# A fused attention and two-MLP kernel: two q tiles and one tile's v windows moved ahead of batch 0's v block rows in the load queue

## The chip, the cores and the metric

The kernel runs on one core of a Trainium2 chip. The metric is device time in microseconds (us), the median of a few runs. TensorE is written PE below (PEld is its weight load), VectorE is DVE, ScalarE is ACT, GpSimd is POOL, and SyncE, which issues almost all loads, is SP (SPq in rows of its queue).

## The reference

For two batches of eight heads, 768 rows and a head width of 64, the reference computes an attention in which every row sees the keys less than 16 rows away and, beside them, one summary key and one summary value for each block of 32 rows (the maximum of the block's keys, the mean of its values). Two MLPs follow on the 1536 x 512 result.

```python
k_sum = k.reshape(B, H, nb, block, D).max(axis=3)
v_sum = v.reshape(B, H, nb, block, D).mean(axis=3)
...
scores_all = np.concatenate([scores_l_m, scores_s], axis=-1)
...
v_all = np.concatenate([v, v_sum], axis=2)
return np.matmul(a, v_all).astype(np.float32)
...
silu = g * (1.0 / (1.0 + np.exp(-g)))
return (silu * val @ w_out).astype(np.float32)
...
h = x @ w_in
g = h - np.tanh(h)
return (g @ w_out).astype(np.float32)
```

## The kernel before

Each engine has one instruction stream written by hand; semaphores tie them together. Nothing is scheduled by a planner, so each engine works strictly in its written order.

Attention goes in tiles of 128 rows, six tiles (0 to 5) for batch 0 and six for batch 1. Batch 0 is done first. For a tile t the loads are: `kn` (the keys, 256 KB), `qn_a` (the queries, 256 KB, three buffers), and `vw_a` (the values, two overlapping windows of 96 rows, 192 KB each, three buffers). Beside them stand the block rows `blk`: all values of a batch, arranged as 96 partitions by 2 halves by 2048 numbers, from which the summary values are made. They are loaded in two halves of 768 KB each (`load_block_half`, L222). Their view of v in DRAM has four groups of heads outermost.

How batch 0 starts: PE transposes the six k tiles and q's tile 0 (`transpose_k`, L444; `transpose_q`, L460), ACT copies them back, DVE takes the block maxima of k (L1003), and PE computes tile 0's scores (`scores`, L485). DVE's written order then is `reduce_half(0)`, `reduce_half(1)`, `shift(A0, 0, 0, ...)`. The two halves are the sums over each block of v (L995, each waits for its half of `blk`); `shift` (L1016) is the step without which ACT cannot take tile 0's exponentials (L799). PE's order is `scores(A0, 0)`, `transpose_q(A0, 1)`, `summary_values` (L530, waits for both halves' sums), six small products that do nothing but keep PE occupied (L646), then the transposes of tile 0's probabilities (L500), tile 1's scores, tile 2's q transpose, and the products of probabilities and values (`weigh_values`, L521).

What comes next in the load queue also depends on that chain: tile 3's value windows reuse tile 0's buffer, so SP waits for `pv_done`, which PE gives at the end of tile 0's second `weigh_values`. Only behind that wait does SP issue batch 1's two halves of `blk`:

```python
for t in range(3, TPB):
    if t == 3:
        load_q0(4)
    load_v0(t)
    if t == 3:
        load_q0(5)
        for hf in range(2):
            load_block_half(1, hf)
    load_k(TPB + t)
```

Batch 1's block rows are added up on POOL (`add_halves`, L388). POOL's first such step stands in its order ahead of `inverse_rms` of tile 2 (L373, L376), which DVE's `scale_x` (L1049), PE's `transpose_x` (L537) and all that follows wait for. After batch 0's attention the MLPs begin (L543 to L545), interleaved with batch 1's attention, and run to the end.

Of the kernel before, what the change touches and what calls it, by code (L numbers as in the profile page):

```python
# [6 lines left out]
def attention_then_two_mlps(nc: bass.Bass, q, k, v, moe_w_gate, moe_w_val, moe_w_out, moe_rms_g,  # L7
# [58 lines left out]
    with ctx:  # L66
# [150 lines left out]
        def _(sp):  # L217
            def load_block_half(g, hf):

                if g:  # L220
                    sp.wait_ge(blk_red, hf + 1)
                sp.dma_start(blk[:, hf, :], v_b[g, hf]).then_inc(blk_in[hf], 16)  # L222

            def load_k(t):

                if t >= TPB:
                    sp.wait_ge(k_T, t - TPB + 1)
                sp.dma_start(kn[t % TPB][:, :].rearrange("p (h d) -> p h d", h=H),  # L228
                             k_v[t // TPB, t % TPB * P:(t % TPB + 1) * P]).then_inc(kn_in[t % TPB], 16)

            def load_windows(dst, src, t, done):
                for w in range(2):
                    sp.dma_start(dst[0:WIN, w, :].rearrange("p (h d) -> p h d", h=H),
                                 src[rows(window_start(t, w), WIN)]).then_inc(done, 16)

            def load_q0(t):
                if t >= 3:
                    sp.wait_ge(q_T, t - 2)
                sp.dma_start(A0.qn[t % 3][:, :].rearrange("p (h d) -> p h d", h=H),
                             q_v[0, t * P:(t + 1) * P]).then_inc(q_in[t % 3], 16)  # L240

            def load_v0(t):
                if t >= 3:
                    sp.wait_ge(pv_done, 2 * (t - 3) + 2)
                load_windows(A0.vw[t % 3], v_v[0], t, vw_in[t % 3])
# [38 lines left out]
            load_q0(0)  # L284
            for t in range(3, TPB):
                load_k(t)
            for hf in range(2):
                load_block_half(0, hf)
            load_q0(1)
            load_v0(0)  # L290
            load_v0(1)
            with nc.allow_non_contiguous_dma(reason="512 single elements, once"):
                sp.dma_start(rms_g[:, :], g_v).then_inc(g_in, 16)
            load_q0(2)
            load_v0(2)
            load_q0(3)
            for t in range(TPB, TPB + 3):
# [693 lines left out]
        def _(dve):  # L991
# [60 lines left out]
            def xT_low(t, src):  # L1052
                dve.wait_ge(xT_hi_done, t + 1)
                (dst, t0), (high, _) = place(xT_lo, t), place(xT_hi, t)
                for c in range(KC):
                    last = nc.vector.scalar_tensor_tensor(  # L1056
                        out=dst[:, c, rows(t0, P)], in0=src[:, c * P:(c + 1) * P], scalar=rms_g[:, c:c + 1],
                        in1=high[:, c, rows(t0, P)].bitcast(f32), op0=ALU.mult, op1=ALU.subtract)
                last.then_inc(xT_lo_done, 1)
# [211 lines left out]
```

## Time and profile before

| what | value |
|---|---|
| time, median of 3 runs | 694.68 us (694.16 to 695.09) |
| span of the profiled execution | 692.5 us |
| time outside the span (median less span) | 2.2 us |
| PE busy | 648.3 us, 94% of the span |
| DVE, ACT, POOL busy | 331.9, 271.8, 31.9 us |
| queue of SP's loads | 49.82 MB |

The time of the profiled execution itself is given only by its span; the span stands 2.2 us under the median of the unprofiled runs, and that difference is taken to lie around the span. A share of busy time is an average over the whole span. The first part, up to about 90 us, is attention with PE often idle, and the rest is the MLPs.

### The profile page before, as it was taken

What the parts mean: (1) busy time and instruction counts of PE and PEld (TensorE: products, weight loads), DVE (VectorE), ACT (ScalarE), POOL (GpSimd) and SP (SyncE); (2) the same over time, 40 slices, a digit from 0 to 9 for tenths busy, and PEclk for the clock granted to TensorE, in tenths of its full rate; (3) what the DMA queues carried; (4) which work ended last, traced back from release to release, by engine and by line L of the source; (5) the groups of instructions that cost most, each with busy time, mean ns of one, the idle gap of its engine ahead of it and who ended that gap; (6) DMA issues with size and microseconds to landing.
All of it is one profiled execution on the core that took longest, in us unless ns stands there. A gap on an engine that the chain in (4) does not pass through costs nothing.

```text
span 692.5 us, 11670 instructions
## 1 busy us (share of the span) xinstructions
PE 648.3 (94%) x4176; PEld 606.3 (88%) x4176; DVE 331.9 (48%) x754; ACT 271.8 (39%) x677; POOL 31.9 (5%) x66
## 2 busy tenths in 40 slices
PE   7273699999999999999999999999999999999997
PEld 7162589999999999999989999999999999989886
DVE  2573775676675323444444445555521254444442
ACT  3184554556454223333333333333311143333332
POOL 2012410001100000000000000000000000000000
PEclk9598799999999999999999999999999999999999
DMA  7674723313431212222222242222203022122202
GB/s 157 139 151 130 180 62 79 75 49 95 98 90 41 61 54 69 72 69 68 65 61 61 61 137 62 67 73 72 76 24 99 1 65 71 62 61 61 61 15 91
DMA packets 105852, 53.34 MB, mean 77 GB/s; under 512 B 46560, under 2 KB 99808, under 8 KB 105440
## 3 DMA queue, kind: packets, MB, share of 16 engines
q1 hardware_dynamic: 104096, 49.82, 27.4%
q10 hardware_dynamic: 1728, 3.15, 1.2%
q8 instruction: 18, 0.29, 0.2%
q14 instruction: 10, 0.08, 0.0%
HBM read 49.81 MB, written 3.15 MB: 76 GB/s over the span
## 4 chain that ended last, share of the span: by engine, by line
PE 85%; DMA 6%; DVE 3%; ACT 2%; SPq 1%; issue 1%; POOL 1%; DVEq 0%; ACTq 0%; POOLq 0%
PE bank L543 20%; PE bank L545 20%; PE bank L544 20%; PE bank L636 6%; PE bank L637 6%; PE bank L635 6%; DMA blk<-in_v_dram 6%; PE bank L521 1%; PE bank L500 1%; SPq L228 1%; ACT xT_hi L817 1%; ACT pr_b L799 1%; POOL blk L388 1%; DVE xT_lo L1056 1%; PE bank L485 1%
## 5 line engine op out<-in xcount | busy, mean ns | idle before, releaser
L543 PE MATMUL bank<-xT_hi,x_hi 128*128 128x384 f32 x448 | 151.6, 338 | 0.6 <-DVE xT_lo L1056 0.6
L545 PE MATMUL bank<-xT_hi,x_lo 128*128 128x384 f32 x448 | 150.2, 335 | 0.0
L544 PE MATMUL bank<-xT_lo,x_hi 128*128 128x384 f32 x448 | 150.2, 335 | 0.0
L1063 DVE TENSOR_TENSOR h_lo<-pd,h_hi 128x384 fp32r<-128x384 f32 (+1 forms) x112 | 62.9, 561 | 70.4 <-ACT h_hi L872 37.1
L543 PEld LDWEIGHTS bank<-xT_hi,x_hi 128*128 128x128 f32 x448 | 84.1, 188 | 3.3 <-DVE xT_lo L1056 0.9
L544 PEld LDWEIGHTS bank<-xT_lo,x_hi 128*128 128x128 f32 x448 | 84.1, 188 | 1.4
L545 PEld LDWEIGHTS bank<-xT_hi,x_lo 128*128 128x128 f32 x448 | 84.1, 188 | 0.0
L637 PE MATMUL bank<-y_hi,h_lo 128*128 128x512 f32 x192 | 76.0, 396 | 0.0
L636 PE MATMUL bank<-y_lo,h_hi 128*128 128x512 f32 x192 | 76.0, 396 | 0.0
L635 PE MATMUL bank<-y_hi,h_hi 128*128 128x512 f32 x192 | 75.9, 395 | 0.0
L1063 DVE TENSOR_TENSOR y_lo<-y_raw,y_hi 128x512 fp32r<-128x512 f32 x56 | 38.5, 688 | 77.3 <-ACT y_hi L832 77.3
L543 PE MATMUL bank<-xT_hi,y_hi 128*128 128x384 f32 x192 | 66.0, 344 | 0.0
L543 PE MATMUL bank<-h_hi,z_hi 128*128 128x384 f32 x192 | 65.2, 340 | 0.0
L544 PE MATMUL bank<-h_lo,z_hi 128*128 128x384 f32 x192 | 65.0, 339 | 0.0
L545 PE MATMUL bank<-h_hi,z_lo 128*128 128x384 f32 x192 | 65.0, 339 | 0.0
L832 ACT CAST y_hi<-y_raw 128x512 fp32r<-128x512 f32 x56 | 34.8, 621 | 75.5 <-PE bank L637 75.5
L545 PE MATMUL bank<-xT_hi,y_lo 128*128 128x384 f32 x192 | 64.3, 335 | 0.0
L544 PE MATMUL bank<-xT_lo,y_hi 128*128 128x384 f32 x192 | 64.2, 334 | 0.0
L856 ACT CAST h_hi<-pd 128x384 f32 (+1 forms) x48 | 24.7, 515 | 94.3 <-DVE pd L1092 94.1
L1118 DVE TENSOR_TENSOR pd<-bank,th 128x384 f32<-128x384 f32 x64 | 35.6, 557 | 30.4 <-ACT th L870 30.4
L872 ACT CAST h_hi<-pd 128x384 fp32r<-128x384 f32 x64 | 32.8, 513 | 40.7 <-DVE pd L1118 40.7
L870 ACT ACTIVATE th<-bank 128x384 f32<-128x384 f32 x64 | 31.4, 491 | 40.8 <-PE bank L545 40.8
(102 smaller groups left out, 903.6 us busy)
## 6 DMA issues: line engine op xcount, KB each, us to landing
x_raw<-in_moe_w_in_dram SPq DMA_DIRECT2D x32, 256.0 KB, 3.0
y_raw<-in_moe_w_out_dram SPq DMA_DIRECT2D x32, 256.0 KB, 2.7
x_raw<-in_moe_w_gate_dram SPq DMA_DIRECT2D x24, 256.0 KB, 3.0
y_raw<-in_moe_w_val_dram SPq DMA_DIRECT2D x24, 256.0 KB, 3.3
z_raw<-in_moe_w_out_dram SPq DMA_DIRECT2D x16, 384.0 KB, 3.4
kn<-in_k_dram SPq DMA_DIRECT2D x12, 256.0 KB, 5.1
blk<-in_v_dram SPq DMA_DIRECT2D x4, 768.0 KB
out_dram<-stage ACTq DMA_DIRECT2D x12, 256.0 KB, 2.5
```

Source lines behind the costliest of these rows:

```text
L543: nc.tensor.matmul(dst, w_hi, a_hi, start=start, stop=False)
L544: nc.tensor.matmul(dst, w_hi, a_lo, start=False, stop=False)
L545: return nc.tensor.matmul(dst, w_lo, a_hi, start=False, stop=stop)
L635: nc.tensor.matmul(AB[t][:], a_hi, w_hi, start=first, stop=False, skip_group_check=True)
L636: nc.tensor.matmul(AB[t][:], a_hi, w_lo, start=False, stop=False, skip_group_check=True)
L637: last = nc.tensor.matmul(AB[t][:], a_lo, w_hi, start=False, stop=final, skip_group_check=True)
L832: nc.scalar.copy(y_hi[:, s, :, :], y_raw[:, s, :, :]).then_inc(y_hi_done, 1)
L856: nc.scalar.copy(dst, pd[:, b, :]).then_inc(h_hi_done, 1)
L870: nc.scalar.activation(th[:, b, :], XB[b][:, 0:NB], ACT.Tanh).then_inc(tanh_done, 1)
L872: nc.scalar.copy(h2_hi[:, s, b, :], pd[:, b, :]).then_inc(h_hi_done, 1)
L1063: nc.vector.tensor_tensor(dst, full, high.bitcast(f32), ALU.subtract).then_inc(done, 1)
L1118: nc.vector.tensor_tensor(pd[:, b, :], XB[b][:, 0:NB], th[:, b, :], ALU.subtract).then_inc(x_bank_free, 1)
```

## The change

Only the order in which SP issues loads at the start changes. q's tile 1, the two windows of v's tile 0 and q's tile 2 were issued behind the two halves of `blk` (q's tile 2 further back still, behind v's tile 1 and the norm weights `rms_g`); they are now issued ahead of them. No load is added, removed or resized, no wait is added, and PE, DVE, ACT and POOL have the same instructions in the same order.

```diff
             load_q0(0)
             for t in range(3, TPB):
                 load_k(t)
+            load_q0(1)
+            load_v0(0)
+            load_q0(2)
             for hf in range(2):
                 load_block_half(0, hf)
-            load_q0(1)
-            load_v0(0)
             load_v0(1)
             with nc.allow_non_contiguous_dma(reason="512 single elements, once"):
                 sp.dma_start(rms_g[:, :], g_v).then_inc(g_in, 16)
-            load_q0(2)
             load_v0(2)
             load_q0(3)
```

This is SP's queue at the start of the program, before. Each row is a run of equal DMA issues, with the tile, its source and the shape.

```order
L239 DMA qn_a<-in_q_dram 128x8x64
L228 DMA kn<-in_k_dram 128x8x64 x3
L222 DMA blk<-in_v_dram 96x1x2048 x2
L239 DMA qn_a<-in_q_dram 128x8x64
L233 DMA vw_a<-in_v_dram 96x8x64 x4
L293 DMA rms_g<-in_moe_rms_g_dram 128x4x1
L239 DMA qn_a<-in_q_dram 128x8x64
L233 DMA vw_a<-in_v_dram 96x8x64 x2
L239 DMA qn_a<-in_q_dram 128x8x64
```

The same place of SP's queue in the changed kernel (one line more in the source moves `rms_g` to L294):

```order
L239 DMA qn_a<-in_q_dram 128x8x64
L228 DMA kn<-in_k_dram 128x8x64 x3
L239 DMA qn_a<-in_q_dram 128x8x64
L233 DMA vw_a<-in_v_dram 96x8x64 x2
L239 DMA qn_a<-in_q_dram 128x8x64
L222 DMA blk<-in_v_dram 96x1x2048 x2
L233 DMA vw_a<-in_v_dram 96x8x64 x2
L294 DMA rms_g<-in_moe_rms_g_dram 128x4x1
L233 DMA vw_a<-in_v_dram 96x8x64 x2
L239 DMA qn_a<-in_q_dram 128x8x64
```

Four more DMAs, 896 KB in all, now stand ahead of the two `blk` halves, and four fewer behind them. Among themselves the moved loads keep their order, and so do those that stayed behind `blk`.

## Rows read from the trace of the kernel before

**Rows 1.** The page: span, TensorE's busy slices, granted clock (40 slices, tenths).

```profile
span 692.5 us, 11670 instructions
...
PE   7273699999999999999999999999999999999997
...
PEclk9598799999999999999999999999999999999999
```

**Rows 2.** Chain that ended last, 0 to 120 us: start, us, what.

```profile
7.34 1.00 SPq L222
8.39 19.51 DMA blk<-in_v_dram
27.93 3.60 DVE redv L995
31.58 1.90 PE bank L530 x8
...
42.63 0.64 PE bank L521 x16
...
44.99 0.98 SPq L222
46.02 19.07 DMA blk<-in_v_dram
65.34 4.47 POOL blk L388
...
73.55 1.09 PE bank L537 x4
```

**Rows 3.** Timeline of DVE, 14 to 35 us; brackets: idle before, and releaser.

```profile
19.56 3.57 DVE L995 TENSOR_REDUCE redv<-blk 96x64 f32<-96x2048 f32 x1 [6.01 <-DMA blk<-in_v_dram]
27.93 3.59 DVE L995 TENSOR_REDUCE redv<-blk 96x64 f32<-96x2048 f32 x1 [4.80 <-DMA blk<-in_v_dram]
31.45 0.27 DVE L1016 CUSTOM_DVE_ANT_0 neg_a<-bank,mask 128x120 f32<-128x120 f32 x1
```

**Rows 4.** Timeline of SP's queue, start and length of the issues.

```profile
9.08 0.47 SPq L239 DMA_DIRECT2D qn_a<-in_q_dram  x1
9.59 19.29 SPq L233 DMA_DIRECT2D vw_a<-in_v_dram  x4
...
30.39 1.85 SPq L233 DMA_DIRECT2D vw_a<-in_v_dram  x2
...
37.30 1.14 SPq L239 DMA_DIRECT2D qn_a<-in_q_dram  x1
```

**Rows 5.** Stretches of 1 us; last columns: clock, DMA share, GB/s.

```profile
5.00:6.00 1.00, 1.00 (x12) 1.00 (x11) 0.00 (x0) 0.00 (x0) 0.66 (x3) 1.00 1.33 235
...
7.00:8.00 1.00, 1.00 (x12) 1.00 (x11) 0.00 (x0) 0.39 (x1) 0.09 (x1) 1.00 1.35 217
...
19.00:20.00 1.00, 0.00 (x0) 0.00 (x0) 0.44 (x1) 0.00 (x0) 0.00 (x0) 0.50 0.26 106
...
34.00:35.00 1.00, 1.00 (x6) 1.00 (x6) 0.00 (x0) 1.00 (x6) 0.00 (x0) 0.50 1.33 171
```

**Rows 6.** Waits up to 110 us (first row); timeline of PE (second row).

```profile
PE bank L460 <- DMA qn_a<-in_q_dram: 14.1, 1, 14.1
```

```profile
29.27 1.09 PE L460 MATMUL bank<-ident,qn_a 128*128 128x128 f32 x4 [14.14 <-DMA qn_a<-in_q_dram]
```

**Rows 7.** Stretches of 0.5 us, columns as in rows 5.

```profile
35.00:35.50 0.50, 0.50 (x6) 0.50 (x5) 0.00 (x0) 0.50 (x4) 0.00 (x0) 0.93 1.38 182
...
72.50:73.00 0.50, 0.00 (x0) 0.00 (x0) 0.50 (x1) 0.00 (x0) 0.50 (x1) 0.50 1.19 323
...
79.00:79.50 0.50, 0.50 (x14) 0.50 (x14) 0.50 (x2) 0.50 (x4) 0.00 (x0) 0.55 0.97 281
```

**Rows 8.** Timeline of PE: the same transposes at full and at half clock.

```profile
54.94 0.65 PE L500 MATMUL bank<-ident,pr_a 128*120 128x128 f32 x4
...
77.72 1.11 PE L500 MATMUL bank<-ident,pr_a 128*120 128x128 f32 x4
```

## The prediction

> **What bounds the kernel now.** I read the page first. PE is busy in nine tenths or more of every slice from the sixth on but the last, and only the first five (87 us) show gaps [rows 1]. So a change in the order of the first loads can act only on those roughly 90 us; afterwards PE has its fixed work, and whatever the start gains or loses arrives at the end unchanged.
>
> Next the chain of work that ended last [rows 2]. The reader is to see two long DMA pieces in it, both `blk`. The first begins with SP's issue at 7.34 us and ends when the second half has landed at 27.9. DVE sums that half in 3.60 us, and at 31.58 PE starts the summary products. From there the chain runs through compute until the end of tile 0's `weigh_values` (42.63 plus 0.64). That releases SP, which issues batch 1's `blk` at 44.99 and 46.0; it lands 19.07 us later. POOL, DVE and PE follow it, and PE is at work again at 73.55. So batch 0's `blk` is on the path, and batch 1's `blk` hangs on it through `pv_done`.
>
> The timeline of DVE shows that nothing can slip around the first piece [rows 3]. DVE sits idle 6.01 us and then 4.80 us, both times for `blk`, and the first `shift` starts at 31.45, right behind the second sum. DVE works in its written order, so `shift` cannot start ahead of the sums, whenever its scores were ready. The waits name one more: PE waited 14.1 us for q's tile 1, until 29.27 [rows 6]. That is the wait which the change addresses. Behind it in PE's order stand the summary products, which could not have started before 31.5 anyway, since they need DVE's second sum. Transposing q's tile 1 takes 1.09 us at the low clock, from 29.27 to 30.36, and leaves 1.2 us of idle time before 31.58 [rows 2, 6]. The wait is real and worth nothing.
>
> Then the DMA side. From 5 to 10 us the channels carry 217 to 235 GB/s (k's last tiles, in 256-byte rows). From 13 to 24 us, while only `blk` moves, they carry about 106 GB/s at a mean busy share of 0.26, against 1.33 before [rows 5]; of eleven rows one stands there, and the others lie within 98 to 115 GB/s. A share of 0.26 of sixteen channels is four channels' worth. So `blk` runs at 1,573 kB / 106 GB/s = 14.8 us for both halves, on about four channels that are full, while the others idle. SP's queue says what lies behind them: q's tile 1 was issued at 9.08 and landed at 29.2, just behind `blk`, and the next issue, v's first window, was held at SP; four window issues took 19.29 us [rows 4]. Loads pass through `blk`'s channels in the order of issue. What is issued ahead of `blk` therefore delays it, by the time those channels need for their share.
>
> **The change part by part.** *Four loads go ahead of blk.* They are 2 x 256 KB of q and 2 x 192 KB of v, 917.5 kB in all. They spread over all the channels as the k tiles do, in the same 256-byte rows, and the queue is full at this point, so their price is time at the saturated rate. By bytes: 917.5 kB at the 217 to 235 GB/s of the k tiles is 4.2 to 3.9 us. By SP's issue time with a full queue: a q tile takes 1.14 us, a pair of v windows 1.85 [rows 4], together 2 x 1.14 + 1.85 = 4.1 us. The two ways agree, and I take 4.1. The bounds come from the fastest and slowest stretch with mixed loads: 323 GB/s gives 2.8 us, 171 GB/s gives 5.4 [rows 5, 7]. Zero is excluded, since those four channels must carry their part of 917.5 kB before they turn to `blk`.
>
> Here a rule of the Trainium skill speaks for a smaller price. The page "DMA: Bandwidth & Descriptors", section Specifications, gives about 358 GB/s as a core's limit from HBM, by which the four loads would be an estimated 2.6 us; the same table says that rows under 512 B do not reach line rate. The trace agrees with the second: these rows are 256 B, and the k loads run at 217 to 235 GB/s [rows 5]. The sum by the first would be 2.6 in place of 4.1.
>
> *blk lands later.* The first half (19.56 us before) would be summed from about 23.7; the sum takes 3.57 us and is over well before the second half, so it stays covered. The second half lands at 27.9 + 4.1 = 32.0, the sum ends at 35.6, and shift, exponentials and summary products all start 4.1 us later. What of that is covered? DVE, PE and ACT have all been idle for `blk`, so nothing.
>
> *What is earlier.* q's tile 1 is transposed and copied at about 13 to 15 us. This takes 1.09 us of PE and an ACT copy out of a place where both were idle: gain 0. v's tile 0 and q's tile 2 are there in time before as well; PE shows no DMA wait other than that one of 14.1 us in the stretch. Gain 0.
>
> *What is later next.* v's tile 1, `rms_g`, v's tile 2, q's tile 3 and batch 1's first three k tiles are issued behind `blk`, as before. Before, the held issues ended at 28.88 and SP finished q's tile 4 at 37.30 + 1.14 = 38.44, then waited until 43.3 for PE [rows 2, 4]. That is 4.8 us of cover. Everything up to there moves by the same 4.1 as `pv_done`, and one q tile less is in it, so the cover stays. If it were gone, batch 1's `blk` would be issued later by what is missing; even both v windows of tile 1 held until `blk` has landed cost only 1.85 of the 4.8.
>
> *Batch 1.* `pv_done` comes at 43.3 + 4.1 = 47.4, and batch 1's `blk`, 19.07 us from issue to landing, lands at 69.2 in place of 65.1. Ahead of it stand the same loads as before (two windows, one q tile), and its own 14.8 us do not change. POOL, DVE, PE follow without slack, PE waiting for them before 73.55. Added here: nothing.
>
> *Sum.* 692.5 + 4.1 = 696.6 us of span; with the 2.2 us outside it, 698.8 us, which is 694.68 + 4.1.
>
> **The clock.** PE's granted clock is 0.50 (1.2 GHz) after the idle time before 29 us and comes back to 1.00 (2.4 GHz) within 35.0 to 35.5, at 0.93 over that stretch, 3.5 us after the summary products began at 31.58. In the second such place work began at 73.55 and the clock was back only in 79.0 to 79.5, 5.9 us later [rows 2, 7]. Before, q's transposes at 29.27 preceded the products; now there is no PE work between about 15 and 35.7 us. If the clock took 5.9 us to return in place of 3.5, 2.4 us of PE work would run at half speed and lose 1.2 us (four transposes take 1.11 in place of 0.65 [rows 8]). I put it at 0 in the sum and keep 1.2 as its upper end.
>
> **The rivals.** *A, the forecast:* the whole chain moves by the time of four loads, 698.8; its own range is 697.5 (2.8 us) to 700.1 (5.4 us). Chance 0.74.
>
> *B, the clock comes back late as well:* 4.1 + 1.2 gives 700.0. For it speaks that PE now starts cold with no work ahead; against it, that the work just ahead of the products was only 1.09 us with a gap behind it. Chance 0.14.
>
> *C, the delay is hidden:* the moved loads pass mostly on the channels that `blk` leaves idle, or the chain behind has slack that the profile does not show, and the time is within 1.4 us of before, about 695.2. For it speaks that twelve channels' worth stands idle from 13 to 24 us; against it, that q's tile 1 landed only behind `blk`, so a part of each load does use `blk`'s channels [rows 4, 6]. Chance 0.08.
>
> *D, faster:* what `blk` suffers from is sharing, and not order. Its halves landed 8.37 us apart (19.56, 27.93) [rows 3], against 7.42 for one half at 106 GB/s. If the v windows let in behind it slowed it, and the four loads cost it nothing, each half would gain 0.95: the place is the landing at 27.9, the price -1.9 us, the time 692.8. It decides only if the four loads cost under 1.9 us, which needs over 480 GB/s where the highest stretch has 323. Chance 0.04.
>
> **How the numbers follow.** A measurement of this kernel can tell about 0.2%, 1.4 us. A and B are slower by more, 0.88 together, of which I leave 0.02 for a price under 1.4 us: slower 0.86. C, with that 0.02, is 0.10 within. D is 0.04 faster. The range takes in A's bounds and B, and widens A's low end slightly for a second half that no longer shares: 697.2 to 701.2. It leaves out C, D and the tails of A and B, somewhat under 2 in 10.
>
> **What would show it.** In the profile of the changed kernel the DVE sum of the second half should start near 32.0 with idle time for `blk` ahead of it, the first `shift` near 35.6, and q's tile 1 transposed by 15 us with its 14.1 us wait gone. `weigh_values` of tile 0 should end near 47.4, batch 1's `blk` be issued near 49.1 and land near 69.2, still about 19 us. The span should be near 696.6. Wrong would be: a second sum that starts under 30 us (rival C or D), a clock that rises later than 3.5 us behind the summary products (B), or `blk` of batch 1 no longer 19 us from issue to landing.

## The result and the profile after

| kernel | median, us | runs | ratio to before, 95% interval |
|---|---|---|---|
| before | 694.85 (694.16 to 695.09) | 4 | |
| changed | 699.05 (698.68 to 699.5) | 4 | 1.0062 (1.0048 to 1.0076) |

The change costs 4.2 us; by the interval it is 3.3 to 5.3. (One run more of the kernel before than in the table of the start moves its median from 694.68 to 694.85.) The profiled execution of the changed kernel took 699.23 us, with a span of 697.4, 4.9 above that of before [rows 1]. In the four runs of the changed kernel the time stands 1.78 to 1.86 us above the span. With the same difference the profiled execution of the kernel before took about 694.3 (an estimate, 692.5 plus 1.8): it was a fast one, half a microsecond under the median, while the changed one lies 0.2 above its own. So 0.7 of the 4.9 is which executions were profiled.

The page of the changed kernel, its span, PE's busy slices and the granted clock:

```profile
span 697.4 us, 11670 instructions
...
PE   8084489999999999999999999999999999999997
...
PEclk9678699999999999999999999999999999999999
```

The gaps of the first five slices are wider in sum, and the sixth now reads 8 in place of 9; from the seventh on the row is as before. SP's queue (start and length of the issues, timeline):

```profile
7.24 1.14 SPq L239 DMA_DIRECT2D qn_a<-in_q_dram  x1
8.43 2.19 SPq L233 DMA_DIRECT2D vw_a<-in_v_dram  x2
10.66 0.84 SPq L239 DMA_DIRECT2D qn_a<-in_q_dram  x1
11.55 1.85 SPq L222 DMA_DIRECT2D blk<-in_v_dram  x2
...
49.70 1.58 SPq L222 DMA_DIRECT2D blk<-in_v_dram  x2
```

The first `blk` issue stands at 11.55 in place of 7.34: 4.2 us for four loads. In that time the queue runs at its full rate, as this stretch shows (the last column is GB/s):

```profile
9.00:10.00 1.00, 1.00 (x11) 1.00 (x10) 0.16 (x1) 0.78 (x2) 0.00 (x0) 1.00 1.35 219
```

The timeline of DVE answers to [rows 3]:

```profile
23.98 3.57 DVE L995 TENSOR_REDUCE redv<-blk 96x64 f32<-96x2048 f32 x1 [8.82 <-DMA blk<-in_v_dram]
31.44 3.57 DVE L995 TENSOR_REDUCE redv<-blk 96x64 f32<-96x2048 f32 x1 [3.89 <-DMA blk<-in_v_dram]
34.92 0.27 DVE L1016 CUSTOM_DVE_ANT_0 neg_a<-bank,mask 128x120 f32<-128x120 f32 x1
```

The first half is summed 4.42 us later, the second 3.51, and `shift` starts 3.47 later. The two halves now lie 7.46 us apart, against 8.37 in [rows 3]. PE's timeline shows q's tile 1 transposed early and what that gave: nothing, since the summary products still wait, now 17.73 us, for DVE.

```profile
16.67 0.66 PE L460 MATMUL bank<-ident,qn_a 128*128 128x128 f32 x4
35.06 1.90 PE L530 MATMUL bank<-redv,ident 96*24 96x128 f32 x8 [17.73 <-DVE redv L995]
```

The chain that ended last, 0 to 125 us (start, us, what), answers to [rows 2]:

```profile
12.76 18.65 DMA blk<-in_v_dram
31.44 3.58 DVE redv L995
35.06 1.90 PE bank L530 x8
...
45.14 1.67 PE bank L485 x32
46.81 1.07 PE bank L521 x16
...
50.42 19.99 DMA blk<-in_v_dram
70.66 4.47 POOL blk L388
...
78.87 1.08 PE bank L537 x4
```

Subtracting [rows 2] from it gives the delay at each place: summary products +3.5, end of tile 0's values (46.81 + 1.07 = 47.88 against 43.27) +4.6, batch 1's `blk` landed +5.3, PE resumes +5.3, and the span +4.9. (After PE resumes, its clock is back 3.9 us later, against 5.9 before, which gives 0.4 back.) Between the first two places lies a second fall of the clock. It comes behind this short wait of PE, and the stretches of half a microsecond show it (columns as in [rows 5]):

```profile
44.05 0.65 PE L500 MATMUL bank<-ident,pr_a 128*120 128x128 f32 x4 [1.77 <-ACT pr_a L799]
```

```profile
38.00:38.50 0.50, 0.50 (x5) 0.50 (x4) 0.00 (x0) 0.50 (x4) 0.00 (x0) 0.56 1.32 220
38.50:39.00 0.50, 0.50 (x7) 0.50 (x6) 0.00 (x0) 0.48 (x4) 0.00 (x0) 1.00 1.28 213
...
45.00:45.50 0.50, 0.50 (x14) 0.43 (x16) 0.50 (x2) 0.50 (x5) 0.00 (x0) 0.76 0.16 33
45.50:46.00 0.50, 0.50 (x19) 0.50 (x15) 0.20 (x1) 0.50 (x3) 0.00 (x0) 0.50 0.00 0
```

The clock came back at 38.4, 3.4 us behind the start of the summary products, as before. Behind 45 it fell to 1.2 GHz again, and tile 2's scores took 1.67 us in the chain and the value products 1.07, against 0.98 and 0.64 before. That is the 1.1 us between +3.5 and +4.6. It is not an effect of the change: the run e10_pool_later below, which has the loads of before and differs from it only from POOL's additions on, shows the same fall. Its PE timeline and one stretch:

```profile
40.05 0.65 PE L500 MATMUL bank<-ident,pr_a 128*120 128x128 f32 x4 [1.77 <-ACT pr_a L799]
```

```profile
41.00:41.50 0.50, 0.50 (x14) 0.44 (x16) 0.50 (x2) 0.50 (x5) 0.00 (x0) 0.78 0.22 50
```

There it takes 14.64 us from the summary products to batch 1's `blk` issue, exactly as in the changed kernel (35.06 to 49.70), against 13.41 in the profile of before. One execution can therefore stand about 1.2 us off another in this stretch, whatever the order of the loads.

### The profile page after: what moved, and what is told of

Its sections match the earlier page's. It is cut to its first block, busy times and chain, and to the rows that moved or that the text cites. A ratio compares the mean times of both kernels' runs of the same rounds, so it can differ in the third digit from the quotient of the medians.

```text
span 697.4 us, 11670 instructions
## 1 busy us (share of the span) xinstructions
PE 650.2 (93%) x4176; PEld 608.1 (87%) x4176; DVE 332.0 (48%) x754; ACT 272.0 (39%) x677; POOL 32.0 (5%) x66
## 4 chain that ended last, share of the span: by engine, by line
PE 84%; DMA 6%; DVE 4%; ACT 2%; SPq 2%; issue 1%; POOL 1%; DVEq 0%; ACTq 0%; POOLq 0%
PE bank L543 20%; PE bank L545 20%; PE bank L544 20%; PE bank L637 6%; PE bank L636 6%; PE bank L635 6%; DMA blk<-in_v_dram 6%; PE bank L521 1%; PE bank L500 1%; SPq L228 1%; ACT xT_hi L817 1%; DVE xT_lo L1056 1%; ACT pr_b L799 1%; PE bank L485 1%; POOL blk L388 1%
## 5 line engine op out<-in xcount | busy, mean ns | idle before, releaser
L1118 DVE TENSOR_TENSOR pd<-bank,th 128x384 f32<-128x384 f32 x64 | 35.7, 557 | 30.5 <-ACT th L870 30.5
```

The lines of the kernel that those rows point to most:

```text
L1118: nc.vector.tensor_tensor(pd[:, b, :], XB[b][:, 0:NB], th[:, b, :], ALU.subtract).then_inc(x_bank_free, 1)
```

## The experiments

All times below are medians, beside runs of the kernel before on the same chip (694.81 us in the first group of four, 694.4 in the second, 694.5 in the third). A run is called by the first part of its label, as e1 for e1_q1_only. A kB is 1000 bytes here, and a KB is 1024, so the 896 KB of the four loads are 917 kB.

**How many bytes stand ahead of blk.** First with q's tile 1 alone moved, against the kernel before:

```diff
             for t in range(3, TPB):
                 load_k(t)
+            load_q0(1)
             for hf in range(2):
                 load_block_half(0, hf)
-            load_q0(1)
             load_v0(0)
```

> Only q's tile 1 (262 kB) goes ahead of blk; everything else stays as before. Theory (bytes ahead of blk delay it, and the whole chain with it): 262 kB at about 223 GB/s is +1.2 us, so about 696.0 us, with the second sum starting near 29.1 and PE's 14.1 us wait for q gone. Rival (removing PE's wait for q is worth something, and the loss of the change comes from the v windows): at or under 694.7 us.

Measured: 696.04 us, ratio 1.0017 (1.0008 to 1.0026). The timeline of DVE in this kernel:

```profile
20.78 3.57 DVE L995 TENSOR_REDUCE redv<-blk 96x64 f32<-96x2048 f32 x1 [7.12 <-DMA blk<-in_v_dram]
29.30 3.57 DVE L995 TENSOR_REDUCE redv<-blk 96x64 f32<-96x2048 f32 x1 [4.95 <-DMA blk<-in_v_dram]
```

The wait for q's tile 1 is gone here too; PE waits for the sum instead, and the kernel is slower by what q's 262 kB cost.

```profile
32.92 1.90 PE L530 MATMUL bank<-redv,ident 96*24 96x128 f32 x8 [17.09 <-DVE redv L995]
```

The clock came back late in this one, at 38.7, 5.8 us behind the summary products.

Then, on top of the changed kernel:

```diff
             load_q0(2)
+            load_v0(1)
             for hf in range(2):
                 load_block_half(0, hf)
-            load_v0(1)
```

> As the changed kernel, and v's tile 1 (two more windows, 393 kB) ahead of blk too. Theory: 1311 kB ahead at about 223 GB/s delays blk by 5.9 us against before, 1.8 us more than the changed kernel, so about 700.8 us. Rival (the loss is a fixed price, for example of the clock coming up late, and not of bytes): the same 699 us as the changed kernel.

Measured: 700.79 us, ratio 1.0083 (1.007 to 1.0097), the second sum at 33.66:

```profile
25.66 3.57 DVE L995 TENSOR_REDUCE redv<-blk 96x64 f32<-96x2048 f32 x1 [10.53 <-DMA blk<-in_v_dram]
33.66 3.57 DVE L995 TENSOR_REDUCE redv<-blk 96x64 f32<-96x2048 f32 x1 [4.42 <-DMA blk<-in_v_dram]
```

Three doses, one price: 262 kB cost 1.23 us, 917 kB 4.20, 1311 kB 5.98, which is 213, 218 and 219 GB/s. The rates agree more closely than the times are known: by the intervals the costs are 0.6 to 1.8, 3.3 to 5.3 and 4.9 to 6.7 us. A fixed price (the rival) is excluded all the same, since the first and the last two don't meet.

**Which channels blk uses.** The order of before, each half in four DMAs of one head group; DVE and POOL wait for four times the count:

```diff
-                sp.dma_start(blk[:, hf, :], v_b[g, hf]).then_inc(blk_in[hf], 16)
+                for c in range(KC):
+                    sp.dma_start(blk[c * NBLK:(c + 1) * NBLK, hf, :], v_b[g, hf, c]).then_inc(blk_in[hf], 16)
```

> The order of before; each half of blk is issued as four DMAs, one for each group of heads, whose outermost dimension is 24 rows in place of 4 groups. Theory (blk fills only four of the sixteen channels because four groups stand outermost, and both blk waits follow from that): by the Trainium skill, page DMA: Bandwidth and Descriptors, section Queues, rings and completion order, the DMAs would use 12 channels; three times 106 GB/s is 318, so both halves take 4.9 in place of 14.8 us, the second sum starts near 18, batch 1's blk lands about 10 us after its issue, and the time falls by 12 to 20 us, to about 677. Rival (the 8 KB rows, or the DRAM layout of v, limit blk to 106 GB/s whatever the channels): no change, 694 to 696.

Measured: 683.24 us, ratio 0.983 (0.9815 to 0.9845): 11.6 us faster. Two stretches of a microsecond in which DVE sums the first half:

```profile
17.00:18.00 1.00, 0.00 (x0) 0.00 (x0) 1.00 (x1) 0.00 (x0) 0.00 (x0) 1.00 0.74 172
18.00:19.00 1.00, 0.00 (x0) 0.00 (x0) 1.00 (x1) 0.00 (x0) 0.00 (x0) 1.00 0.65 156
```

The busy share is 0.65 to 0.74 in place of 0.26 [rows 5], and 40 of the 64 packets of these two microseconds, with nearly all the bytes, are 8 KB rows of `blk`. So the number of channels was what held `blk` back, and the rival (8 KB rows or the layout in DRAM) falls. The gain missed the forecast of about 677 us: the stretches carry 156 to 172 GB/s, and not 318. Spread over twelve channels (a share of 0.74 is about twelve sixteenths), each moves 13 to 14 GB/s, where each of the four moved 26.5. In the chain of this kernel batch 1's `blk` is again a long piece:

```profile
20.81 3.61 DVE redv L996
...
42.63 11.97 DMA blk<-in_v_dram
54.85 4.47 POOL blk L389
```

The second sum starts at 20.81 in place of 27.93; batch 1's last issue-to-landing piece is 11.97 us in place of 19.07. That piece is for the last of eight DMAs; from the first issue (39.33) to POOL's start it is 15.5 us in place of 20.3, and not the 10 of the forecast. Why a channel is slower there (the 24 partitions that each DMA writes, or the other loads among them) was not taken apart.

The same edit in the changed order:

> The changed order, with blk issued by groups of heads as in e4_blk_by_head (683.2 us in the order of before). Theory (the price of the change is the channel time of the 917 kB ahead of blk, whoever is behind them; sums and shift still wait for blk): about 4 us slower than e4, 686 to 688 us. Rival (the loss was there only because blk filled four channels to the brim; with blk spread out the four loads cost about nothing, and q's tile 1 being early pays): within 1 us of e4.

Measured: 687.51 us, ratio 0.9897 (0.9882 to 0.9912). Its DVE timeline:

```profile
21.11 3.57 DVE L996 TENSOR_REDUCE redv<-blk 96x64 f32<-96x2048 f32 x1 [6.20 <-DMA blk<-in_v_dram]
25.35 3.57 DVE L996 TENSOR_REDUCE redv<-blk 96x64 f32<-96x2048 f32 x1 [0.67 <-DMA blk<-in_v_dram]
```

The second sum starts 4.5 us later than with `blk` spread in the order of before, and the time is 4.3 higher. The price of the four loads does not depend on `blk` filling its channels.

**What the clock costs.** On the changed kernel:

```diff
+            keep_clock_up(100)
             summary_values(A0, A0.OB[1])
             keep_clock_up(6)
```

> As the changed kernel, and PE gets 100 more small dummy products while it would sit idle for blk (about 14 us of idle time at 0.14 us each), so that its clock does not fall before the summary products. Theory (the clock is a side effect of the wait, worth one to two us in either order and no part of the order's price): the summary products take 1.0 in place of 1.9 us and the time is 697.3 to 698.5. Rival (the low clock caused most of the change's loss): back to about 695.

Measured: 700.53 us, ratio 1.0084 (1.007 to 1.0098). This run answers nothing about the loss: each of the 100 dummy products took 0.22 us (two entries of the timeline each) in place of the 0.14 assumed, and PE was still at them when the sum was ready at 35.7. The summary products, in this kernel's PE timeline:

```profile
16.81 22.50 PE L646 MATMUL bank<-ident 128*128 128x128 f32 x200
39.24 1.05 PE L530 MATMUL bank<-redv,ident 96*24 96x128 f32 x8
```

With 60 dummy products:

> As e3_clock_kept with 60 in place of 100 calls. There 200 small products took 22.5 us and held PE until 39.2, past the end of blk's sum near 35.1, so it showed nothing of the clock. 120 products take 13.5 us and end near 30.8, before the sum. Theory: the summary products run at full clock (1.0 or 1.05 us in place of 1.90), the clock costs 1 to 2 us of the changed kernel's time, not its difference to before; 697.0 to 698.3 us. Rival (the low clock explains the change's loss): about 695. Second rival (ACT's exponentials bound this place and PE's clock is hidden): 699.

Measured: 698.63 us, ratio 1.0061 (1.0047 to 1.0075). PE's timeline:

```profile
16.64 13.56 PE L646 MATMUL bank<-ident 128*128 128x128 f32 x120
35.15 1.90 PE L530 MATMUL bank<-redv,ident 96*24 96x128 f32 x8 [4.95 <-DVE redv L996]
```

PE was idle for 4.95 us again, and the summary products took 1.90 as without the dummy work. So a third:

> As e6_clock_kept_60 with 78 calls. There PE was done with its dummy products at 30.2, stood idle 4.95 us until the sum, and the summary products still took 1.90 us: the clock had fallen again, so the run did not test it. 156 products end near 34.2, 0.9 us ahead of the sum. Theory: the summary products take 1.05 us, and the low clock costs the changed kernel 1 to 2 us: 697.0 to 698.3. Rival (ACT's exponentials bound this place): 698.6 to 699.

Measured: 697.69 us (696.63 to 699.23), ratio 1.0042 (1.0029 to 1.0054). PE's timeline:

```profile
16.35 17.58 PE L646 MATMUL bank<-ident 128*128 128x128 f32 x156
35.71 1.05 PE L530 MATMUL bank<-redv,ident 96*24 96x128 f32 x8 [1.77 <-DVE redv L996]
36.69 2.90 PE L646 MATMUL bank<-ident 128*128 128x128 f32 x12
39.39 0.98 PE L500 MATMUL bank<-ident,pr_a 128*120 128x128 f32 x4
```

The summary products now run at full clock, and the ratio is 0.2% below the changed kernel's, 1.4 us; the two intervals still overlap (1.0029 to 1.0054 and 1.0048 to 1.0076), so the size of this gain, and strictly that there is one, is not shown. But the clock fell right behind them (the small products take 2.90 us, the transposes 0.98), so a partly kept clock was measured, not the whole of its price, and the spread of this kernel's runs is the widest of all. With the products at full clock 3.2 us of loss against the kernel before remain, which itself had them at 1.90 us. That speaks against the clock as the cause of the loss. The same dummy products in the order of before, which would compare like with like, were not run; that the loss is one of bytes rests on the three doses.

**What the early loads could be good for.** The change brings q's tiles 1 and 2 and v's tile 0 while `blk` is on its way, but DVE and PE have the sums first in their orders. This edit puts tile 0's and tile 1's work ahead of them (on ACT, `copy_summary_values` moves behind tile 1's first exponentials likewise):

```diff
 # PE
-            summary_values(A0, A0.OB[1])
             keep_clock_up(6)
...
                 transpose_probs(A0, t, 1)
+                if t == 0:
+                    summary_values(A0, A0.OB[1])
                 weigh_values(A0, t, 0)
 # DVE
-            reduce_half(0)
-            reduce_half(1)
             shift(A0, 0, 0, mask_of(0))
...
                 copy_probs(A0, t, 1)
+                if t == 0:
+                    reduce_half(0)
+                    reduce_half(1)
```

> The changed load order, and the two sums over blk move on DVE behind tile 0's and tile 1's shift, the summary products on PE behind both transposes of tile 0's probabilities, and the copy of the summary on ACT behind tile 1's first exponentials. Theory (the early q and v loads were worthless only because DVE's and PE's orders put the sums first): tile 0's exponentials and tile 1's scores are done while blk is on its way; the end of tile 0's values, 47.9 in the changed kernel, comes at about 42.6, and the time falls by about 5 us to 694. Rival (all of it is bound by blk and what follows it anyway): 698 to 699.

Measured: 694.74 us, ratio 1.0006 (0.9997 to 1.0015). PE's timeline:

```profile
19.28 1.05 PE L485 MATMUL bank<-kwin_a,qT_a 64*64 64x120 f32 x32
20.26 0.66 PE L460 MATMUL bank<-ident,qn_a 128*128 128x128 f32 x4
...
35.44 1.90 PE L530 MATMUL bank<-redv,ident 96*24 96x128 f32 x8 [14.09 <-DVE redv L996]
...
43.35 0.73 PE L521 MATMUL bank<-vw_a,prT_a 120*64 120x64 f32 x16
```

Tile 1's scores and q's tile 2 are done by 21, and tile 0's values end at 44.1 in place of 47.9. The gain is 4.3 us, a little under the 5 of the forecast (the values were to end at 42.6), and it only makes up for the loss. PE ran at the low clock until 43.5 here, 8.0 us behind the start of its summary products, which may be the rest. The same reordering with the loads of before:

> The same reordering of DVE, PE and ACT as e7_sums_behind_tile0, with the load order of before, in which q's tile 1 lands behind blk at 29.2 us and q's tile 2 at about 35. Theory: the sums now wait on DVE for tile 1's scores and these for q's tiles 1 and 2, so that the sums end near 43 in place of 31.5; 703 to 707 us, about 10 us above e7. Rival (the load order does not matter to this kernel beyond the bytes ahead of blk): 4 us below e7, about 690.

Measured: 704.08 us, ratio 1.0137 (1.0122 to 1.0153). PE waited for q's tile 1 and then for tile 2, and DVE's sums, now behind them, started at 36.10:

```profile
28.41 1.09 PE L460 MATMUL bank<-ident,qn_a 128*128 128x128 f32 x4 [13.28 <-DMA qn_a<-in_q_dram]
...
34.39 0.63 PE L460 MATMUL bank<-ident,qn_a 128*128 128x128 f32 x4 [1.04 <-DMA qn_a<-in_q_dram]
...
43.20 1.90 PE L530 MATMUL bank<-redv,ident 96*24 96x128 f32 x8 [7.74 <-DVE redv L996]
```

So the order of the change is worth 9.3 us to this arrangement of the engines and costs 4.2 us in the old one. Whether q's tile 1 is waited for says nothing; whether something useful stands behind it does.

**Towards a faster kernel.** The reordering of e7 and the split of `blk` together, in the changed order:

> The changed load order, with both the reordering of e7_sums_behind_tile0 and blk issued by groups of heads as in e5_blk_by_head_after (687.5 us). Theory: e7's gain of 4.3 us shrinks, since blk's second half now lands at 25.4 and the work that e7 puts in its shadow still fits there: 683 to 684 us. Rival (with blk spread out the sums are early enough and tile 0's work delays them): 687 or more.

Measured: 683.31 us, ratio 0.9837 (0.9823 to 0.9851). That is 4.2 below the changed order with `blk` spread, and equal to the order of before with it (683.24): with `blk` spread, the change and the reordering together give nothing over the order of before. Then the second `blk` wait, in the order of before: POOL's `add_halves(1)` moves from `t == 1` to `t == 3` of its loop, the other levels from `t == 2` to `t == 4`.

> The order of before; only POOL's additions over batch 1's blk move behind the inverse roots of tile 3 and tile 4, so that nothing of batch 0 waits for batch 1's blk by POOL. Theory (the second blk wait reaches PE through POOL's order, but v's tile 4 windows, queued behind blk on the same channels, land at about 66 and are next): PE resumes near 67 in place of 73.5, and the time falls by 4 to 8 us, to about 689. Rival (POOL's wait is the only one): 680 or less. Second rival (something else of the load queue binds at the same place): 694.

Measured: 691.13 us, ratio 0.9953 (0.9938 to 0.9967), 3.4 faster, a little less than forecast. PE's timeline (first row) and the waits of 40 to 100 us (second row) show who is next:

```profile
68.86 1.12 PE L521 MATMUL bank<-vw_a,prT_a 120*64 120x64 f32 x16 [7.53 <-issue]
```

```profile
ACT x_hi L826 <- DMA x_raw<-in_moe_w_gate_dram: 9.4, 1, 9.4
```

PE stands idle 7.53 us for tile 4's values, and ACT 9.4 us for the first MLP weights, all queued behind `blk`. The releaser of PE's wait is not named, but the trace shows it. The second of tile 4's v windows was issued at 60.44 and landed 8.3 us later, at 68.7, just ahead of PE's 68.86, and the other two things that PE waits for at this step (the copied probabilities and the emptied bank) were done by 62.6. All three together, in the changed order:

> The changed load order with the reorderings of e9_both and e10_pool_later together. Theory: both blk waits are short and the sums are in the shadow of loads: 676 to 680 us. Rival (the load queue as a whole is now the bound, so POOL's order gives nothing more): as e9_both.

Measured: 680.78 us, ratio 0.9802 (0.9787 to 0.9816), just outside the forecast of 676 to 680. It is the fastest version, 13.7 us under before; most of that, 11.6 us, is the split of `blk` alone. The split with POOL's later additions in the order of before was not run, so it is not shown that the fastest version needs the changed order.

## Why the prediction was right

The forecast of 698.8 us was rival A's mechanism: the chain moves by the channel time of the four loads. The measured 699.05 lies 0.25 from it, closer than the interval of 3.3 to 5.3 us can vouch for. The mechanism is shown, the last quarter of a microsecond is luck. By its steps:

*The wait for q's tile 1 is worth nothing.* Shown: with that load alone ahead of `blk` the wait is gone and the kernel is 1.2 us slower.

*Bytes ahead of blk at the saturated rate, 4.1 us.* Shown by three doses at 213 to 219 GB/s; and SP's four issues took 4.2 us at 219 GB/s. Here the Trainium skill's page "DMA: Bandwidth & Descriptors" (section Specifications) would have given an estimated 2.6 us by its limit from HBM; the runs decide for the rate of 256-byte rows, in agreement with its line on rows under 512 B.

*The landing of the second half.* In the two profiled executions it came 3.5 us later, not 4.1. That is scatter. Four other kernels have the changed order of loads up to there (e3, e6, e12 and e7), and their second sums start at 31.53 to 32.03, with the changed kernel's 31.44 a mean of 31.77; e10 has the order of before, and it starts at 27.40, with the 27.93 of before a mean of 27.67. The difference of the means is 4.1 us, the term of the sum. The first half came 4.8 later by the same means.

*Rival D.* The halves do lie closer in the changed order: 7.4 to 7.7 us apart in the five kernels, against 8.3 and 8.4 in the two. But it is the first half that comes later than the price of the loads, and the second pays that price in full. D's saving did not appear. What keeps the first half back was not taken apart.

*The chain behind it is rigid.* Right to about a microsecond: tile 0's values ended at 47.9 (forecast 47.4), batch 1's `blk` was issued at 49.7 (49.1) and landed at 70.4 (69.2). The profiled execution added 1.1 us between the summary products and the end of tile 0's values, by the second fall of the clock, and 0.6 us from batch 1's first `blk` issue to the start of POOL's additions (49.70 to 70.63, against 44.99 to 65.31). Of the other kernels with `blk` unsplit seven show 20.3 to 20.5 us for the latter and one, e8, 20.9, so I take it for scatter of one execution. So the +4.9 of the profiles is the sum of this pair: 3.5, 1.1 and 0.6, less the 0.4 that the clock gave back behind 78.87.

*The time outside the span.* The recorded executions show 1.8 us, not 2.2: the prediction set a median against the span of an execution faster than the median. The forecast time is not touched, since it is also 694.68 + 4.1. The span should have been forecast as 697.0 in place of 696.6; the changed kernel's runs have 696.9 to 697.7.

*The clock comes back late (rival B).* Not in the changed kernel, where it came back 3.4 us behind the start of the summary products, against 3.5 before and 3.4 in e10. But it came late in three kernels that also have loads ahead of `blk`: 5.8 us in e1, 4.5 in e2, 5.6 in e6. The stretch from the summary products to batch 1's `blk` issue took 14.5, 13.9 and 14.3 us there, against 13.4 and 14.6 in before and e10. With `blk` spread it came late in both orders, 6.7 us in e4 (the order of before) and 5.5 in e5. So a late return does happen, but not in the changed order alone, and its price of about 1 us is no larger than what one execution differs from another. Whether the changed order makes it likelier is open. The fall at 45 us is another event, and the order of before has it too. The prediction put the clock at 0 in the sum; no run here asks for another value.

*The loss is hidden (rival C).* Excluded here, and with `blk` spread over more channels too, where the change costs 4.3 us.

*About four channels carry blk.* Shown by the busy share of 0.65 to 0.74 once its DMAs have 24 rows outermost. By the same page of the Trainium skill, section Why a DMA increments its semaphore by 16 and not by 1 (the expectation of e4 names another section), a DMA uses the largest number up to 16 that divides the outermost sizes of both sides. That is 4 before and 12 in the split, and the shares agree (0.26 and at most 0.74 of sixteen). What went wrong in that experiment's forecast was to give each of twelve channels the rate of each of four.

## What to carry to other kernels

A wait that an engine spends on a load is worth removing only if what stands behind it in that engine's order can run; look at the next instruction's releaser before moving the load. Loads ahead of the one that the chain waits for cost their bytes at the rate of a full queue; here the trace of before gave 4.1 us for what measured 4.2 (3.3 to 5.3). Don't read a difference under a microsecond or so from two single profiles: look for the same instruction in other kernels that have the same program up to there. A busy share far below one while a single load is in flight says that the load uses few channels: look at its outermost dimension before its place in the queue.

## What the runs showed of the hardware

PE's granted clock fell to 0.50 behind 45 us in the changed kernel while PE was at work; ahead of that PE had been idle from 42.3 to 44.05, 1.77 us. In e10 it fell likewise at 41.3, behind an idle time of 1.77 us up to 40.05. In the kernel before PE was idle 1.71 us at the same step of its program, in e12 1.70, and the clock stayed at 1.00. So nearly the same idle time at the same step ended either way, and the fall cost 1.1 us of the chain. Behind the start of the summary products the clock came back after 3.4 to 3.5 us in before, changed and e10, after 4.5 to 6.7 us in e1, e2, e4, e5 and e6, and after 8.0 us in e7.

`blk` moved at 26.5 GB/s on each of four channels (106 GB/s in all) and at 13 to 14 on each of twelve (156 to 172 GB/s in all), in the same 8 KB rows.
